# Causal scores computed in quarters of the TensorE array, with half of every second chunk of keys and values turned, and one output copy moved to VectorE

## What is computed

```python
def _attn_ref(q, k, v):                     # 2 x 8 heads, 768 tokens, 64 wide
    gamma = 1.0 - 2.0 ** (-5.0 - np.arange(H, dtype=np.float32))
    for t in range(S):
        state = gamma[None, :, None, None] * state + np.einsum('bhd,bhe->bhde', k[:, :, t], v[:, :, t])
        y[:, :, t] = scale * np.einsum('bhd,bhde->bhe', q[:, :, t], state)
```

## Time and profile before

| | |
|---|---|
| median of 3 runs | 448.47 us (448.3 to 448.62) |
| the profiled execution | 448.04 us, of which the span from the first to the last instruction is 446.3 us |
| TensorE | busy 439.8 us, 99% of the span; granted clock 0.999 of full speed |
| VectorE, ScalarE, GpSimd | busy 317.1, 227.1 and 290.1 us |
| retention layer | from the start to about 55 us |

### The profile page before, as it was taken

The page is one execution under the profiler, slowest core; times in us unless marked ns, Lnnn a source line. Parts: engine busy times, 40 slices in busy tenths (PEclk is TensorE's granted clock), DMA queues, the critical chain, the costliest instruction groups (busy, mean ns, idle before and its releaser), DMA issues.

```text
span 446.3 us, 8371 instructions
## 1 busy us (share of the span) xinstructions
PE 439.8 (99%) x2958; PEld 399.4 (89%) x2958; DVE 317.1 (71%) x669; ACT 227.1 (51%) x530; POOL 290.1 (65%) x390
## 2 busy tenths in 40 slices
PE   7999999999999999999999999999999999999997
PEld 6898998989898899898988989888999999999886
DVE  3564889767876857786686677648557888887963
ACT  3458865532451465444245234214436777777853
POOL 3856745989788699997886696632703355566650
PEclk9999999999999999999999999999999999999999
DMA  9999304221321211321122260020153534333214
GB/s 222 246 232 293 104 1 141 60 82 49 94 55 53 85 46 50 94 94 49 52 91 80 63 166 0 1 47 2 31 141 79 143 89 102 96 84 98 90 48 165
DMA packets 68473, 41.50 MB, mean 93 GB/s; under 512 B 35792, under 2 KB 62672, under 8 KB 68432
## 3 DMA queue, kind: packets, MB, share of 16 engines
q1 hardware_dynamic: 66288, 40.37, 33.2%
q10 hardware_dynamic: 2144, 0.60, 0.6%
HBM read 28.37 MB, written 3.15 MB: 71 GB/s over the span
## 4 chain that ended last, share of the span: by engine, by line
PE 96%; ACT 1%; DVE 1%; issue 1%; POOL 0%; POOLq 0%; DVEq 0%
PE ps L980 30%; PE ps L961 25%; PE ps L1096 8%; PE ps L1115 4%; PE ps L1149 4%; PE ps L1130 4%; PE ps L1066 4%; PE ps L1185 3%; PE ps L821 3%; PE ps L833 3%; PE ps L811 2%; PE ps L920 2%; PE ps L846 1%; PE ps L872 1%; PE ps L878 1%
## 5 line engine op out<-in xcount | busy, mean ns | idle before, releaser
L1378 ACT ACTIVATE h_t_hi<-ps 128x384 fp32r<-128x384 f32 x64 | 31.3, 490 | 126.2 <-DVE ps L1732 68.2
L980 PE MATMUL ps<-w_hi,h_t_lo 128*128 128x512 f32 x192 | 76.1, 397 | 0.0
L980 PE MATMUL ps<-w_lo,h_t_hi 128*128 128x512 f32 x192 | 75.8, 395 | 0.0
L980 PE MATMUL ps<-w_hi,h_t_hi 128*128 128x512 f32 x192 | 74.7, 389 | 0.0
L680 POOL TENSOR_TENSOR w_lo<-raw_w,w_hi 128x512 fp32r<-128x512 f32 x32 | 43.1, 1370 | 40.9 <-ACT w_hi L1327 30.3
L771 POOL TENSOR_SCALAR a<-a,inv_den,weight 128x768 f32<-128x768 f32 (+5 forms) x48 | 34.0, 717 | 53.2 <-DVE inv_den L1970 28.6
L1713 DVE SCALAR_TENSOR_TENSOR h_t_lo<-ps,h_t_hi 128x384 fp32r<-128x384 f32 x64 | 35.6, 557 | 32.6 <-ACT h_t_hi L1378 32.6
L665 POOL TENSOR_TENSOR w_lo<-w_sum,w_hi 128x256 fp32r<-128x256 f32 x60 | 44.4, 750 | 2.4
L980 PEld LDWEIGHTS ps<-w_hi,h_t_lo 128*128 128x128 f32 x192 | 36.0, 187 | 7.7
L1466 ACT ACTIVATE a<-a,neg_max 128x768 f32<-128x768 f32 (+5 forms) x48 | 32.2, 674 | 17.1 <-DVE neg_max L1951 17.1
L961 PE MATMUL ps<-xq_T_lo,w_hi 128*128 128x384 f32 x120 | 40.5, 338 | 0.0
(11 more groups left out here) (200 smaller groups left out, 1189.1 us busy)
## 6 DMA issues: line engine op xcount, KB each, us to landing
raw_w<-in_moe_w_ch SPq DMA_DIRECT2D x64, 256.0 KB, 2.9
k_twice_hi<-pj_hi SPq DMA_DIRECT2D x32, 96.0 KB, 2.2
k_twice_lo<-pj_lo SPq DMA_DIRECT2D x32, 96.0 KB, 2.2
out_y<-out_sb SPq DMA_DIRECT2D x11, 256.0 KB, 2.0
raw_k<-in_k SPq DMA_DIRECT2D x7, 384.0 KB, 5.4
raw_q<-in_q SPq DMA_DIRECT2D x7, 384.0 KB, 5.9
raw_v<-in_v SPq DMA_DIRECT2D x7, 384.0 KB, 5.4
q_both<-pj_hi SPq DMA_DIRECT2D x16, 96.0 KB, 2.1
```

The source lines that it names most:

```text
L980: mm = pe.matmul(acc_bank(tau), h_tile(a_, m, which)[:, u * P:(u + 1) * P], w2[b_][:, m % 2, part, :], start=(m % NG == 0 and which in ("1 ...
L1378: act.activation(h_tile("hi", m, part), part_bank(m, part), ACT.Relu).then_inc(s_hhi, 1)
```

## The change: what it does

1. **Scores in quarters** (pairs 1 to 7; pair 0 is as before). A chunk's 128 keys are taken as two halves of 64. In an even chunk, the lower half of the keys (partitions 0 to 63) is multiplied with all 128 queries, and the upper half only with the queries 64 to 127; the 64 by 64 square of later keys and earlier queries isn't computed. The mask puts zeros there as before.
2. **Odd chunks are turned**: their keys and values are loaded with the two halves of 64 tokens exchanged, so that the half with 128 queries lies in partitions 64 to 127. The decay table of the keys and the mask follow (`causal` has four chunks' masks instead of one; pair 0 gets an unturned slot in the table). A load of keys or values is therefore three transfers instead of one.
3. **VectorE copies part 0 of the outputs** of pairs 0 to 5 (`first_out`), behind `states`; ScalarE keeps part 1 of all, and both parts of pairs 6 and 7.
4. **ScalarE's and VectorE's work around it is moved**: all four `weight_hi(0, ...)` stand in iteration 6 (two of them were in 5), `scale_w1(1)` moves from 6 to 7, and `weight_hi(1, ...)` stands behind it; of the four `centre(0, 0, kk)` of iteration 6, two move to iteration 7, ahead of its `states`.

```diff
+    of_k = 1.0 / power
+    of_k[1::2] = np.roll(of_k[1::2], P // 2, axis=1)
...
-        causal = sb(ctx, "causal", [P, P])
+        causal = sb(ctx, "causal", [P, 4, P])
...
+        def wait_copied(engine, it, g):
+
+            if it >= NIT - 2:
+                engine.wait_ge(s_yx, NIT - 2 + LAST_OUT.index((it, g)) + 1)
+            elif g == 1:
+                engine.wait_ge(s_yx, it + 1)
+            else:
+                engine.wait_ge(s_yx0, it + 1)
...
+        def load_even_chunks(engine, n, it):
+
+            to = raw[n][:, it % RB].rearrange("p j (c r) d -> p (j c) r d", r=2)
+            return engine.dma_start(to[:, :, 0], by_turns[n][0][it])
+
+        def load_odd_chunks(engine, n, it, half):
+
+            to = raw[n][:, it % RB].rearrange("p j (c r) d -> p (j c) r d", r=2)
+            return engine.dma_start(to[head_rows(half), :, 1], by_turns[n][1][it][head_rows(1 - half)])
...
+                if n == "q":
+                    load_q(sp, it).then_inc(s_load[n][it % RB], 16)
+                else:
+                    load_even_chunks(sp, n, it).then_inc(s_load[n][it % RB], 16)
+                    for half in range(2):
+                        load_odd_chunks(sp, n, it, half).then_inc(s_load[n][it % RB], 16)
...
+            def later_tokens(c, half):
+
+                start = head_rows(half if c % 2 == 0 else 1 - half).start
+                pool.affine_select(out=causal[head_rows(half), c, :], in_=causal[head_rows(half), c, :],
+                                   compare_op=ALU.is_ge, fill=0.0, base=-start, pattern=[[1, P]],
+                                   channel_multiplier=-1).then_inc(s_const, 1)
...
-                for c in range(G):
-                    for j in range(2):
-                        rows = slice(j * D, (j + 1) * D)
-                        mm = pe.matmul(s_bank(g)[:, j, c], k_t(G * g + c)[rows], q_slot(it)[rows, G * g + c, :],
-                                       start=True, stop=True)
+                for c in range(G * g, G * g + G):
+                    if it == 0:
...
+                    else:
+                        for half in (c % 2, 1 - c % 2):
+                            seen = slice(0 if half == c % 2 else D, P)
+                            for j in range(2):
+                                mm = pe.matmul(s_bank(g)[head_rows(half), j, c % G, seen], k_t(c)[head_rows(j), head_rows(half)],
+                                               q_slot(it)[head_rows(j), c, seen], start=True, stop=True,
+                                               skip_group_check=True)
                 mm.then_inc(s_s, 1)
...
                 for unit in range(4):
                     turned(it, unit)
-                if it == NIT - 1:
-                    weight_hi(1, "A11")
-                    weight_hi(1, "A12")
                 if it != 2:
-                    for g in range(2):
-                        y_out(max(0, it - 2), g)
+                    y_out(max(0, it - 2), 1)
                 if it == HP:
                     act.wait_ge(s_gcol, 16)
                 if it == HP + 1:
                     scale_w1(0)
-                    for name in FIRST_WEIGHTS[:2]:
+                if it == HP + 2:
+                    for name in FIRST_WEIGHTS:
                         weight_hi(0, name)
-                if it == HP + 2:
-                    for name in FIRST_WEIGHTS[2:]:
-                        weight_hi(0, name)
+                if it == NIT - 1:
                     scale_w1(1)
+                    weight_hi(1, "A11")
+                    weight_hi(1, "A12")
...
+            def first_out(it):
+
+                dve.wait_ge(s_y, y_turn(it, 0) + 1)
+                dve.tensor_copy(x[:, it, part_of(0), :], y_bank(it, 0).rearrange("p (c t) -> p c t", c=G)).then_inc(s_yx0, 1)
...
+            dve.wait_ge(s_const, 11)
             for it in range(1, NIT):
                 apply_causal(it, 0)
                 apply_causal(it, 1)
                 b, kk = divmod(it - 2, HP)
                 if it >= 2 and kk > 0:
                     first_sum(b, kk)
-                if it == HP + 2:
-                    for kk in range(KT):
-                        centre(0, 0, kk)
+                if it in (HP + 2, HP + 3):
+                    for kk in range(2):
+                        centre(0, 0, 2 * (it - HP - 2) + kk)
                 states(it)
+                if it < NIT - 1:
+                    first_out(it - 1)
```

More of the change, by code:

```diff
@@ L46, in decay_tables @@
     of_q = power.reshape(2, P, seq // P // 2, heads).transpose(0, 2, 1, 3).reshape(power.shape)
-    both = np.stack([of_q / np.sqrt(head_dim), 1.0 / power])
+    of_k = 1.0 / power
+    of_k[1::2] = np.roll(of_k[1::2], P // 2, axis=1)
+    both = np.stack([of_q / np.sqrt(head_dim), of_k])
     both = both.reshape(2, seq // P, P, heads // 2, 2).transpose(2, 0, 3, 1, 4)
-    return both.reshape(P, 2, heads // 2, -1).astype(np.float32)
+    first = both[:, :, 0:1].copy()
+    first[:, 1, 0] = (1.0 / power)[:, :, 0:2].transpose(1, 0, 2)
+    return np.concatenate([first, both], axis=2).reshape(P, 2, heads // 2 + 1, -1).astype(np.float32)
 class Chain:
@@ L96, in retention_moe_program @@
     heads = {n: a.rearrange("b (i j) (c p) d -> (b i) p j c d", j=2, p=P) for n, a in (("k", k), ("v", v))}
+    by_turns = {n: a.rearrange("b (i j) (c r p) d -> r (b i) p (j c) d", j=2, r=2, p=P) for n, a in (("k", k), ("v", v))}
     q_rows = q.rearrange("b (i j) (g p t) d -> (b i) p (j g) (t d)", j=2, p=P, t=G)
@@ L630, in _ @@
             diagonal(ident)
-            pool.memset(causal[:, :], 1.0).then_inc(s_const, 1)
+            pool.memset(causal[:, :, :], 1.0).then_inc(s_const, 1)
             pool.wait_ge(s_const, 3)
-            pool.affine_select(out=causal[:, :], in_=causal[:, :], compare_op=ALU.is_ge, fill=0.0, base=0,
-                               pattern=[[1, P]], channel_multiplier=-1).then_inc(s_const, 1)
+            def later_tokens(c, half):
[3 more added lines that the diff above has]
+                                   channel_multiplier=-1).then_inc(s_const, 1)
+            for c in range(4):
+                for half in range(2):
+                    later_tokens(c, half)
+            pool.wait_ge(s_const, 11)
             pool.tensor_scalar(mean_of[:, :], ident[:, :], 0.0, 1.0 / DM, ALU.mult, ALU.add).then_inc(s_const, 1)
             pool.memset(masked[:, :, :], 0.0).then_inc(s_const, 1)
-            pool.wait_ge(s_const, 6)
+            pool.wait_ge(s_const, 13)
             pool.affine_select(out=masked[:, NC - 1, :], in_=masked[:, NC - 1, :], compare_op=ALU.is_ge, fill=MASKED, base=0,
```

43 lines of the change are left out of this document (22 added, 21 removed).

## The result

The changed kernel takes **452.59 us** (median of 4 runs, 451.9 to 453.4) against 448.38 of the kernel before on the same chip: ratio 1.0094, interval 1.0077 to 1.0112. It is slower by 4.2 us where 1.85 us less were forecast. Its profiled execution took 452.66, with a span of 450.6 against 446.3.

A forecast was written before the change was run, and what follows sets the result against it. The prediction took TensorE's own pace to bound the retention stage, with full transfers close behind. Scores 2.8 us earlier less 0.95 for a longer way out gave 1.85: from the median 448.47 to 446.6 us, range 445.6 to 448.7.

The forecast's parts named there:

- The scores' block: TensorE from last state pair to chunk outputs: 1.75 to 1.23 us, 0.52 gained; iteration 7's scores 2.8 earlier in all.
- The transfers: Loads of keys and values in three transfers each: taken to cost nothing, with 0.3 us left at pair 6's values.
- The way out: From iteration 7's scores to the second mean and part "22": 0.9 to 1.0 us longer through the moved work.
- T: Start of iteration 7's first mask on VectorE, from which the forecast counted the times after it.
- VectorE's copy at nothing: VectorE's new copy of part 0, 0.5 us, hides where VectorE waits for the next scores; no cost.
- GpSimd's last queries: In iteration 6 GpSimd splits weights ahead of the last queries; no wait forecast, with 0.6 us to spare.
- The supply binds: Rival: loads or GpSimd's last queries 0.7 to 1.6 us late, less 0.3 lost; 447.0 to 447.9, chance 0.16.
- The column halves take turns: Rival: two quarters of one row half can't run at once; four blocks 2.25 instead of 1.75, 452.5 us, chance 0.07.
- Quarters in step: Rival: a 64-column pass takes as long as one of 128; block 1.53, gain 0.22, 448.4 us, chance 0.17.

The follow-up runs named there:

- the supply mended: Changed kernel with all moves undone; ScalarE issues the keys' odd chunks, those of pairs 2 and 3 behind its first copies, pair 1's by SyncE: 446.28 us, 0.9961.
- unturned quarters: Kernel before with the scores of pairs 1 to 7 in quarters but no chunk turned, loads and everything else as before: 447.02 us, 0.9964.
- the kernel with GpSimd held: Unturned quarters with all the moves, plus a wait that starts GpSimd's second-group weight splits only after VectorE's low part of B12: 453.96 us, 1.0125.

## Why the prediction was wrong

- **The scores' block: right in mechanism, a little too large.** The iteration became 5.38 instead of the forecast 5.34 (5.86 - 0.52), and the block 1.26 instead of 1.23. From iteration 1's scores to iteration 5's the profile has 34.86 - 14.63 = 20.23, before 36.37 - 14.57 = 21.80: 1.6 gained of the 1.8 that the step has up to there. With the supply mended, the whole way to iteration 7 is 32.46 (47.24 - 14.78) against 34.35: 1.9 instead of 2.8. Iteration 1 gains nothing there, since pair 2 comes no sooner (18.85 - 14.78 = 4.07 against 3.99); iteration 2 gives 0.40 and iterations 3 and 4 give 0.42 each; iterations 5 and 6 together give 0.7 where 1.0 was added up for them. In iterations 3 and 4 0.06 is missing against the changed kernel: the chunk outputs take 1.39 to the next row instead of 1.36 and the key-values 0.71 instead of 0.68, as in the other turned kernels in which ScalarE copies both parts; why isn't explained.
- **The transfers: the first step that failed.** "I take nothing, since the queue and not SP sets the pace now." It set the pace before the change, with one transfer for each load. Three take SyncE 1.8 to 1.9 us, more than the 1.5 that the queue needs for 384 KB at the 255 GB/s of the earlier trace rows (an estimate), and the share fell to 0.92. The sum over an iteration wouldn't have warned me: seven transfers are 4.2 us and with two of weights 5.4, beside an iteration of 5.38 and beside 4.6 us that the queue needs for the three loads of a pair at 255 GB/s. What the profiled execution shows instead is the order in time: SyncE stands behind a full queue for two halves (3.04), and the loads behind them then leave late and one at a time. And I looked at the values of pair 6, while those of pair 5 were late: before, they were issued at 31.84 and there 4.6 us later, at 36.4, 2.9 ahead of their key-values (39.26). They came 3.3 later, and TensorE 1.6 sooner. In the profiled execution the wait is 2.10 and the fall of the clock behind it 1.55, of the 4.35 by which iteration 7's scores miss the forecast. In finished times, 2.1 us come back when ScalarE issues eight of the transfers.
- **The way out, the second step that failed: "0.9 to 1.0 us longer"; it was 3.0.** The term is what ScalarE's moved weights add: "That adds 0.1". They add 2.1: in the profile of the change with these weights back, part "22" starts 61.16 - 48.68 = 12.48 us behind the scores, 0.85 more than before, against 14.60. The places came as forecast: ScalarE's copies end at T + 6.7 (T + 6.9 forecast), VectorE starts the head sums at T + 6.33 (T + 6.3), with T = 51.35. What was missing is the length of VectorE's rows when GpSimd works beside them: I took 1.21 for the head sums and they last 1.99, and two low parts add 0.5 and 1.05. The forecast followed ScalarE's moved scaling to ScalarE's own work and not to GpSimd, which waits for it and does its sums and splits later. Measured as finished time, the moved weights are 2.5 us in the changed kernel and 3.1 with unturned quarters.
- **VectorE's copy at nothing:** 0.6 in the finished time, at the edge of what can be told. **GpSimd's last queries** were in time; no row of TensorE waits for them in iteration 6.
- **The rivals.** *The supply binds* named one of the two causes, and its price, loads 0.7 to 1.6 late less 0.3, was too low: the profiled execution has 2.10 of wait, and the fall of the clock behind it was left out. *The column halves take turns* (452.5) meets the number and is refuted by the rows: 1.26 us for the block (29.47 to 30.73) where it would be 2.25. The number is met by chance. *Quarters in step* (a block of 1.53) is refuted by the same rows. The unturned cut comes to 1.51 (29.76 to 31.27 in its trace), since one column half has all the long matmuls. The range ended at 448.7, since I priced both the supply and the way out too low and had no case in which both go wrong.

## What to carry to other kernels

Before a load is cut into several, set the time that its parts take to issue against the time that the queue needs for its bytes; that the queue is full now says nothing about it. A sum over an iteration that just fits isn't enough, since the issuing engine also stands behind a full queue at times. Look at every load with little slack, not at one. When work is moved on one engine, follow who waits for its result: here a scaling moved by one iteration carried another engine's work into the critical stretch, where the two slow each other in operations with both inputs in SBUF. And when a step makes the bounding engine faster, ask what supplies it at the new pace, with its own price for a wait: here the clock fell behind one of 2.10 us. When a kernel's executions spread over 3 us, one profile is one of them; the granted clock of the others says whether it is like them.

## What the runs showed of the hardware

- Quarters of 64 by 64 with passes of 128 and 64 columns mixed don't go in step: balanced three and three, six chunks take 1.17 to the next shape, six and six 1.45, whole halves 1.54. Scores also start before the state outputs of the same shape have ended (34.72 in the changed kernel, between two of their records).
- After a wait of 2.10 us the granted clock was 0.56 over the next 3.73 us. After one of 1.27 at the same place (the change with ScalarE's weights back, key-values at 39.24) it stayed at 1.00. After one of 2.71 in the kernel with GpSimd held it was 0.51 over 6.20 us.
- The time to issue goes by transfers more than by bytes: a 96 KB one over 64 partitions takes the issuing engine 0.64 us, a 192 KB one over 128 partitions 0.51 to 0.62, a 384 KB one of values 0.51 (before, 25.12). Behind a full queue (a share of 0.98) two of 96 KB took 3.04.
- VectorE's operations on 384 columns with both inputs in SBUF take 0.6 alone and 1.0 beside GpSimd, those on 768 columns 0.95 alone and 1.5 to 2.0; the subtractions, with one input in PSUM, take 1.94 and 1.95 either way.
